# Attention and two MLPs on one core: the first matrix of each MLP by one level of Strassen, one MLP after the other

## The chip, the cores and the metric

The kernel runs on one core of a Trainium2 chip. The metric is the device time of one execution in microseconds (us). Three runs of the kernel before gave 1108.28, 1108.68 and 1110.57 us; the median is 1108.68.

## What is computed

All arrays are fp32. q, k and v are [1, 6016, 256].

```python
qn = q / (norm(q, axis=1) + 1e-6);  kn = k / (norm(k, axis=1) + 1e-6)
s = kn.transpose(0, 2, 1) @ qn / tau          # 256 x 256
a = softmax(s, axis=-1)
x = (v @ a).reshape(6016, 256)
h = x @ w_in                                  # 256 -> 2048, first MLP
x2 = (h * sigmoid(1.702 * h)) @ w_out         # 2048 -> 256
h = x2 @ w2_in                                # 256 -> 2048, second MLP
out = (maximum(h, 0) + alpha * minimum(h, 0)) @ w2_out
```

## The kernel before

Every fp32 product is made of three fp32r matmuls (`split_product`, L307 to L310): the high part of the weights by the high part of the data, high by low, and low by high. The high part is a rounded copy, which ScalarE writes; the low part is the fp32 value less the high one, which VectorE writes (L618), and at the start GpSimd too (L295 to L302).

The attention stage (to about 52 us) streams q and k, sums their squares, forms the 256 x 256 softmax, and folds it into the first matrix of the first MLP: W1P, eight pieces of 512 columns and six matmuls (L435 to L439). v then goes straight into the first MLP.

The MLPs work on the transposed data: features on partitions, tokens along the free axis. There are twelve token tiles, one of 384 tokens and eleven of 512, and for each a pass "A" (first MLP) and a pass "B" (second MLP). A pass has 16 chunks f of 128 hidden features. In each, `first_product` (L312) makes one bank of h from six matmuls, over two halves of 128 input features, and `second_product` (L333) adds six matmuls into two banks of output sums, two chunks later (LAG = 2). `phase_steps` (L352) writes this order out by hand; the passes go A0, A1, B0, A2, then nine turns of a hardware loop with B and A, then B10, B11. A whole tile is thus carried through both MLPs, and x2 never leaves the core.

Between the two matmul groups of a chunk stand, in "A", ScalarE's two activations out of PSUM (L474 to g, L477 to g_hi) and VectorE's low part (L618); in "B", two VectorE operations (L634 and L638, the leaky ReLU), ScalarE's rounding (L482) and the low part. v tiles come by DMA in blocks of 32 x 32 and are transposed by VectorE (L655), which also transposes the results (L680).

## Time and profile before

| | |
|---|---|
| median of 3 runs | 1108.68 us |
| span of the profiled execution | 1106.9 us |
| TensorE busy | 1098.3 us, 4937 matmuls |
| VectorE busy | 623.9 us, 954 instructions |
| ScalarE busy | 405.2 us, 715 instructions |
| GpSimd busy | 29.4 us, 28 instructions |
| granted clock of TensorE | 1.000 |

All times are of one profiled execution; its span is from the first to the last instruction, and the time of an execution holds a little before and after it. Matmuls are pipelined: one is shown with some 0.39 us, but the next starts 0.23 us later, so rates are read from start to start. "Idle before" names what released an engine after it had waited.

### The profile page before, as it was taken

How to read it: one execution, taken by the hardware profiler on the slowest of the kernel's cores; microseconds unless marked ns; L12 is line 12 of the kernel's file. 1: busy time of each engine (PE TensorE's matmuls, PEld its weight loads, DVE VectorE, ACT ScalarE, POOL GpSimd, SP SyncE). 2: the span in 40 equal slices, each digit the busy share in tenths (PEclk: the TensorE clock that was granted, in tenths of full speed). 3: DMA queues.
4: the chain of work that ended last, by engine and by line, in shares of the span. 5: the costliest groups of instructions: out<-in, count | busy, mean ns of one | idle time of the engine just before them, and what ended most of it. 6: DMA issues, size and time to landing. Idle time of an engine off the chain costs nothing.

```text
span 1106.9 us, 13843 instructions
## 1 busy us (share of the span) xinstructions
PE 1098.3 (99%) x4937; PEld 912.6 (82%) x4937; DVE 623.9 (56%) x954; ACT 405.2 (37%) x715; POOL 29.4 (3%) x28
## 2 busy tenths in 40 slices
PE   9999999999999999999999999999999999999998
PEld 8899898888888888888888888888888888888886
DVE  6974474275276257258348437527626725834775
ACT  6785523323323323322432432332332332343221
POOL 4500000000000000000000000000000000000000
PEclk9999999999999999999999999999999999999999
DMA  8742000010010110110100100001001011010011
GB/s 338 271 118 77 0 1 15 1 20 10 10 20 0 19 19 0 19 19 0 19 14 5 19 5 14 14 5 19 5 14 19 0 19 19 0 19 0 1 20 20
DMA packets 108536, 33.37 MB, mean 30 GB/s; under 512 B 100048, under 2 KB 104672, under 8 KB 108256
## 3 DMA queue, kind: packets, MB, share of 16 engines
q1 hardware_dynamic: 30368, 23.34, 6.7%
q10 hardware_dynamic: 78144, 9.71, 5.7%
q8 instruction: 15, 0.25, 0.1%
q14 instruction: 9, 0.07, 0.0%
HBM read 26.88 MB, written 6.16 MB: 30 GB/s over the span
## 4 chain that ended last, share of the span: by engine, by line
PE 98%; DMA 1%; DVE 0%; SPq 0%; ACT 0%; issue 0%
PE ps L308 32%; PE ps L309 32%; PE ps L310 32%; PE ps L401 2%; DMA q_sb<-q_dram 1%; PE ps L435 0%; PE ps L439 0%; PE ps L436 0%; DVE inv_norm L732 0%; SPq L259 0%; DVE sim L735 0%; SPq L260 0%; DVE neg_max L737 0%; DVE out_sb L680 0%; ACT sim L539 0%
## 5 line engine op out<-in xcount | busy, mean ns | idle before, releaser
L618 DVE TENSOR_TENSOR g_lo<-g,g_hi 128x512 fp32r<-128x512 f32 (+1 forms) x384 | 259.6, 676 | 341.0 <-ACT g_hi L477 331.2
L482 ACT ACTIVATE g_hi<-g 128x512 fp32r<-128x512 f32 (+1 forms) x192 | 119.7, 623 | 400.4 <-DVE g L638 400.4
L474 ACT ACTIVATE g<-ps 128x512 f32<-128x512 f32 (+1 forms) x192 | 113.1, 589 | 275.9 <-PE ps L310 275.9
L634 DVE TENSOR_SCALAR neg_part<-ps,alpha_T 128x512 f32<-128x512 f32 (+1 forms) x192 | 141.9, 739 | 125.4 <-PE ps L310 125.4
L308 PE MATMUL ps<-g_hi,w1o_hi 128*128 128x512 f32 (+1 forms) x384 | 150.1, 391 | 0.0
L309 PE MATMUL ps<-g_lo,w1o_hi 128*128 128x512 f32 (+1 forms) x384 | 150.1, 391 | 0.0
L310 PE MATMUL ps<-g_hi,w1o_lo 128*128 128x512 f32 (+1 forms) x384 | 150.0, 391 | 0.0
L308 PE MATMUL ps<-g_hi,w2o_hi 128*128 128x512 f32 (+1 forms) x384 | 148.0, 385 | 0.0
L309 PE MATMUL ps<-g_lo,w2o_hi 128*128 128x512 f32 (+1 forms) x384 | 147.9, 385 | 0.0
L310 PE MATMUL ps<-g_hi,w2o_lo 128*128 128x512 f32 (+1 forms) x384 | 147.9, 385 | 0.0
L308 PE MATMUL ps<-vT_hi,w1i_hi 128*128 128x512 f32 (+1 forms) x352 | 136.8, 389 | 0.0
L309 PE MATMUL ps<-vT_lo,w1i_hi 128*128 128x512 f32 (+1 forms) x352 | 136.7, 388 | 0.0
L310 PE MATMUL ps<-x_hi,w2i_lo 128*128 128x512 f32 (+1 forms) x352 | 135.5, 385 | 0.0
L310 PE MATMUL ps<-vT_hi,w1i_lo 128*128 128x512 f32 (+1 forms) x352 | 135.4, 385 | 0.0
L309 PE MATMUL ps<-x_lo,w2i_hi 128*128 128x512 f32 (+1 forms) x352 | 135.3, 384 | 0.0
L308 PE MATMUL ps<-x_hi,w2i_hi 128*128 128x512 f32 (+1 forms) x352 | 135.2, 384 | 0.0
L638 DVE SCALAR_TENSOR_TENSOR g<-ps,neg_part 128x512 f32<-128x512 f32 (+1 forms) x192 | 129.4, 674 | 0.4
L477 ACT ACTIVATE g_hi<-ps 128x512 fp32r<-128x512 f32 (+1 forms) x192 | 112.2, 584 | 0.0
L310 PEld LDWEIGHTS ps<-g_hi,w1o_lo 128*128 128x128 f32 x384 | 72.1, 188 | 16.1
L308 PEld LDWEIGHTS ps<-g_hi,w1o_hi 128*128 128x128 f32 x384 | 72.1, 188 | 15.7
L309 PEld LDWEIGHTS ps<-g_lo,w1o_hi 128*128 128x128 f32 x384 | 72.1, 188 | 15.2
L308 PEld LDWEIGHTS ps<-g_hi,w2o_hi 128*128 128x128 f32 x384 | 72.1, 188 | 14.6 <-DVE g_lo L618 0.4
(106 smaller groups left out, 1053.3 us busy)
## 6 DMA issues: line engine op xcount, KB each, us to landing
k_sb<-k_dram SPq DMA_DIRECT2D x10, 512.0 KB, 11.5
q_sb<-q_dram SPq DMA_DIRECT2D x10, 512.0 KB, 13.2
out_dram<-out_sb ACTq DMA_DIRECT2D x76, 64.0 KB, 1.9
v_raw<-v_dram ACTq DMA_DIRECT2D x72, 64.0 KB, 2.0
stage<-w_in_dram SPq DMA_DIRECT2D x4, 512.0 KB, 13.5
w1o_raw<-w_out_dram SPq DMA_DIRECT2D x1, 2048.0 KB, 8.6
stage<-w_in_dram SPq DMA_DIRECT2D x1, 2048.0 KB, 9.2
stage<-w_out_dram SPq DMA_DIRECT2D x1, 2048.0 KB, 8.3
```

The costliest lines, as they stand in the source:

```text
L308: nc.tensor.matmul(into, w_hi_ap, x_hi_ap, start=first, stop=False)
L309: nc.tensor.matmul(into, w_hi_ap, x_lo_ap, start=False, stop=False)
L310: return nc.tensor.matmul(into, w_lo_ap, x_hi_ap, start=False, stop=last)
L401: last = nc.tensor.matmul(ps[:, m, 0:C], k_sb[:, j, m * P:(m + 1) * P], q_sb[:, j, :], start=(j == 0), stop=False)
L474: nc.scalar.activation(g[:, f % 2, 0:n], ps[:, H + f % NH, 0:n], ACT.Gelu_apprx_sigmoid)
L477: nc.scalar.activation(g_hi[:, f % NG, 0:n], ps[:, H + f % NH, 0:n], ACT.Gelu_apprx_sigmoid).then_inc(hi_ready, 1)
L482: nc.scalar.activation(g_hi[:, f % NG, 0:n], g[:, f % 2, 0:n], ACT.Copy).then_inc(hi_ready, 1)
L618: return nc.vector.tensor_tensor(lo, full, hi.bitcast(fp32), ALU.subtract)
L634: nc.vector.tensor_scalar(neg_part[:, f % 2, 0:n], h, 0.0, alpha_T[:, f:f + 1], ALU.min, ALU.mult).then_inc(neg_done, 1)
L638: nc.vector.scalar_tensor_tensor(out=g[:, f % 2, 0:n], in0=h, scalar=0.0, in1=neg_part[:, f % 2, 0:n], op0=ALU.max, op1=ALU.add).then_inc( ...
```

## The change

The first product of each MLP is computed by the Winograd form of Strassen's scheme. A step n takes two token blocks (of 448 tokens in the first pair, of 512 in the other five) and two chunks of 128 hidden features, with two halves of the input features: a 2 x 2 by 2 x 2 block product, in seven products of three matmuls in place of eight. Weights and data enter as seven combinations each (`wi_hi`, `wi_lo`, `x_hi`, `x_lo`): four of them are sums, made by GpSimd (`wide_tops`, `wi_tops`, `tops_1` to `tops_4`; for the first two chunks of weights by VectorE). Products 1, 6, 7 and 4 add up in one bank, and ScalarE copies the bank to SBUF (`keep`) after each of the first three; VectorE's `sum_block` adds these copies to the banks of products 2, 5 and 3 and gives the blocks G11, G22 and G12; G21 is the bank itself. The second product of step n-1 is issued within step n, in four runs of six matmuls, in the order that `turn_order` gives, into four banks of sums.

A pair of blocks has 8 steps, an MLP has 48, and both have 96. The whole first MLP comes first; its result is copied out (`take_out`) and stored in a DRAM tensor, x2_stash, and loaded again for the second MLP, whose weights take the place of the first's during steps 41 to 52. The activations now read blocks of fp32 in SBUF (G21 from PSUM); in the second MLP ScalarE makes the negated part with ReLU, and VectorE adds it with the factor 1 - alpha (`leak`). All stores go by the queue of SP. The program has no hardware loops. The attention stage is as before, but all of W1P comes ahead of the first step, ScalarE alone takes it out of PSUM, and it is made into sums and split afterwards.

```diff
+    PAIRS = -(-N // (2 * W))
+    FIRST = (N - (PAIRS - 1) * 2 * W) // 2
+    QUADS = NF // 2
+    LAYER = PAIRS * QUADS
+    STEPS = 2 * LAYER
...
+        PRODUCT = {1: (0, 0), 2: (1, 5), 3: (6, 2), 4: (2, 6), 5: (3, 1), 6: (4, 3), 7: (5, 4)}
...
+        B11, T1, B22, T2, T3, B21, T4 = range(TOPS)
+        G11, G12, G21, G22 = range(4)
+        BLOCK = {G11: (0, 0), G12: (0, 1), G21: (1, 0), G22: (1, 1)}
...
+            return (G11, G21, G22, G12) if n % QUADS in (0, QUADS - 1) else (G11, G22, G21, G12)
...
+                if LAYER - QUADS <= n < LAYER:
+                    if s > 0:
+                        sp.wait_ge(wi_low, s)
+                    else:
+                        sp.wait_ge(wide_low, NFB - 1)
+                    for h in range(KC):
+                        sp.dma_start(wi_raw[:, 0:8:A21, :] if h == 0 else wi_raw[:, 1:3, :], w2i_v[h, s]).then_inc(wi_in, 16)
+                if LAYER - 4 <= n < LAYER - 4 + QUADS:
+                    s = n - (LAYER - 4)
+                    sp.wait_ge(wo_low, QUADS + s - 1)
+                    sp.dma_start(wo_raw[:, s % 2], w2o_v[s]).then_inc(wo_in[s % 2], 16)
...
+            for fb in range(NFB):
+                pool.wait_ge(w0_high, fb * KC + 2)
+                cols = slice(fb * BANK, (fb + 1) * BANK)
+                minus(w0_lo[:, 1, cols], stage[:, 1, cols], w0_hi[:, 1, cols].bitcast(fp32)).then_inc(w0_pool, 1)
+                if fb == 1:
+                    tops_1(0)
+                if fb == 2:
+                    tops_23(0)
+                    tops_4(0)
...
+            def wide_lows(fb):
+                pool.wait_ge(wide_high, fb + 1)
+                s = slice(2 * fb, 2 * fb + 2)
+                minus(wi_lo[:, s], wide[:, fb, :, 0:TOPS, :], wi_hi[:, s].bitcast(fp32)).then_inc(wide_low, 1)
+            wide_tops(1)
+            wide_lows(1)
...
+            def top(product, n, bank, first):
+                nt, s, gp = width(n), n % QUADS, pair(n)
+                w, x = PRODUCT[product]
+                if s == 0:
+                    pe.wait_ge(x_low, TOPS * gp + x + 1)
+                into = ps[:, bank, 0:nt]
+                xh, xl = x_hi[gp % 2][:, x, 0:nt], x_lo[gp % 2][:, x, 0:nt]
+                nc.tensor.matmul(into, wi_hi[:, s, w, :], xh, start=first, stop=False, skip_group_check=True)
+                nc.tensor.matmul(into, wi_hi[:, s, w, :], xl, start=False, stop=False, skip_group_check=True)
+                nc.tensor.matmul(into, wi_lo[:, s, w, :], xh, start=False, stop=True,
+                                 skip_group_check=True).then_inc(p_done[product], 1)
...
+            def second(n, begin, end):
...
+                order = turn_order(n)
+                for m in range(begin, end):
+                    b = order[m // 6]
+                    c, kind = divmod(m % 6, 3)
+                    i, t = BLOCK[b]
+                    f = 2 * s + i
+                    if m == 0 and n % LAYER < QUADS:
+                        pe.wait_ge(wo_low, layer(n) * QUADS + s + 1)
+                    if m % 6 == 0:
+                        pe.wait_ge(g_low[b], n + 1)
+                    opens = s == 0 and b in (G11, G22)
+                    if opens and kind == 0 and gp > 0:
+                        pe.wait_ge(y_out, 4 * (gp - 1) + 2 * t + c + 1)
+                    closes = s == QUADS - 1 and b in (G21, G12)
...
+                    done = nc.tensor.matmul(ps[:, 2 * t + c, 0:nt], wl if kind == 2 else wh, (g_lo if kind == 1 else g_hi)[:, b, 0:nt],
+                                            start=opens and kind == 0, stop=closes and kind == 2, skip_group_check=True)
+                    if m % 6 == 5:
+                        done.then_inc(y_used[b], 1)
+                    elif closes and m % 6 == 2:
+                        done.then_inc(y_half, 1)
...
+            def step(n):
+                if n < STEPS:
+                    if n >= 2:
+                        pe.wait_ge((acted if layer(n - 2) == 0 else leaky)[G21], n - 1 - LAYER * layer(n - 2))
...
+                    top(1, n, Y(n), True)
+                if n > 0:
+                    second(n - 1, 0, 6)
+                    pe.wait_ge(c_ready[G22], n)
+                    top(3, n - 1, Z, False)
+                if n < STEPS:
+                    pe.wait_ge(p1_kept, n + 1)
+                    top(6, n, Y(n), False)
+                if n > 0:
+                    second(n - 1, 6, 12)
+                if n < STEPS:
+                    if n > 0:
+                        pe.wait_ge(c_ready[G11], n)
+                    top(2, n, X, True)
+                    pe.wait_ge(u2_kept, n + 1)
+                    top(7, n, Y(n), False)
+                if n > 0:
+                    second(n - 1, 12, 18)
+                if n < STEPS:
+                    if n > 0:
+                        pe.wait_ge(c_ready[G12], n)
+                    top(5, n, Z, True)
+                    pe.wait_ge(u3_kept, n + 1)
+                    top(4, n, Y(n), False)
+                if n > 0:
+                    second(n - 1, 18, 24)
...
+            widen(0)
+            widen(1)
+            x_part(0, B11)
+            split_w0(3)
+            x_part(0, T1)
+            widen(2)
+            widen(3)
+            wide_part(0)
+            x_part(0, B22)
+            x_part(0, T2)
+            widen(4)
+            widen(5)
+            x_part(0, T3)
+            x_part(0, B21)
+            widen(6)
+            widen(7)
+            x_part(0, T4)
+            load_table(ACT.Gelu_apprx_sigmoid)
+            wo_part(0)
...
+            for n in range(STEPS + 1):
+                gp, s = pair(n) + 1, n % QUADS
+                if n < STEPS:
+                    keep(n, 0, 1, p1_kept)
+                if n > 0:
+                    high(n - 1, G21)
+                    activate(n - 1, G12)
+                if n < STEPS:
+                    keep(n, 1, 6, u2_kept)
+                if n > 0:
+                    high(n - 1, G12)
+                if n == STEPS:
+                    continue
+                if n in (0, 2, 3):
+                    wide_part({0: 1, 2: 2, 3: 3}[n])
+                if LAYER - 6 <= n < LAYER - 6 + QUADS:
+                    wi_part(n - (LAYER - 6))
...
+                activate(n, G11)
+                keep(n, 2, 7, u3_kept)
+                high(n, G11)
...
+                if LAYER - 3 <= n < LAYER - 3 + QUADS:
+                    wo_part(n + 3)
+                activate(n, G22)
+                activate(n, G21)
+                high(n, G22)
...
+            def sum_block(n, b):
...
+                product, bank, kept = {G11: (2, X, 0), G22: (5, Z, 2), G12: (3, Z, 1)}[b]
+                dve.wait_ge(p_done[product], n + 1)
+                dve.wait_ge({G11: p1_kept, G22: u3_kept, G12: u2_kept}[b], n + 1)
+                nc.vector.tensor_tensor(g[:, b, 0:nt], part[:, kept, 0:nt], ps[:, bank, 0:nt], ALU.add).then_inc(c_ready[b], 1)
...
+            for n in range(STEPS + 2):
+                gp, s = pair(n) + 1, n % QUADS
+                if s == 1 and n > 1:
+                    take_out(gp - 2, 1, 0)
+                    take_out(gp - 2, 1, 1)
+                if n == STEPS + 1:
+                    continue
+                if n > 0:
+                    low_block(n - 1, G22)
+                    sum_block(n - 1, G12)
+                    if layer(n - 1) == 1:
+                        low_block(n - 1, G21)
+                        leak(n - 1, G12)
+                    else:
+                        low_block(n - 1, G21)
+                if n < STEPS:
+                    sum_block(n, G11)
+                if n > 0:
+                    low_block(n - 1, G12)
+                if n < STEPS:
+                    if layer(n) == 1:
+                        leak(n, G11)
...
+                    if n < QUADS - 1:
...
+                    if LAYER - 3 <= n < LAYER - 3 + QUADS:
...
+                    sum_block(n, G22)
+                    low_block(n, G11)
...
+                    if layer(n) == 1:
+                        leak(n, G22)
+                        leak(n, G21)
+                if s == 0 and n > 0:
+                    take_out(gp - 2, 0, 0)
+                    take_out(gp - 2, 0, 1)
```

## Rows read from the trace of the kernel before

**Rows 1.** The page: busy shares, the chain; then whom TensorE waited for.
```profile
PE 1098.3 (99%) x4937; PEld 912.6 (82%) x4937; DVE 623.9 (56%) x954; ACT 405.2 (37%) x715; POOL 29.4 (3%) x28
...
PE 98%; DMA 1%; DVE 0%; SPq 0%; ACT 0%; issue 0%
...
PE ps L401 <- DMA q_sb<-q_dram: 1.6, 1, 1.6
PE ps L378 <- POOL ones L288: 1.1, 1, 1.1
PE ps L422 <- ACT sim L539: 0.8, 2, 0.4
```

**Rows 2.** The timeline of TensorE (start, us, operation) where passes begin.
```profile
138.99 0.33 PE L308 MATMUL ps<-x_hi,w2i_hi 128*128 128x384 f32 x1
...
173.05 0.39 PE L308 MATMUL ps<-vT_hi,w1i_hi 128*128 128x512 f32 x1
...
348.68 0.39 PE L308 MATMUL ps<-vT_hi,w1i_hi 128*128 128x512 f32 x1
...
393.19 0.39 PE L308 MATMUL ps<-x_hi,w2i_hi 128*128 128x512 f32 x1
...
436.84 0.39 PE L308 MATMUL ps<-vT_hi,w1i_hi 128*128 128x512 f32 x1
```

**Rows 3.** The timeline of single operations in steady passes, and one low part's wake.
```profile
501.64 0.39 PE L310 MATMUL ps<-x_hi,w2i_lo 128*128 128x512 f32 x1
502.07 0.75 DVE L634 TENSOR_SCALAR neg_part<-ps,alpha_T 128x512 f32<-128x512 f32 x1 [0.77 <-PE ps L310]
...
509.57 0.63 ACT L482 ACTIVATE g_hi<-g 128x512 fp32r<-128x512 f32 x1 [2.09 <-DVE g L638]
510.11 1.14 ACT L495 ACTIVATE vT_hi<-v_turn 128x512 fp32r<-128x512 f32 x2
...
1059.00 0.68 DVE L618 TENSOR_TENSOR g_lo<-g,g_hi 128x512 fp32r<-128x512 f32 x1
1059.60 0.68 DVE L638 SCALAR_TENSOR_TENSOR g<-ps,neg_part 128x512 f32<-128x512 f32 x1
...
1098.62 0.69 DVE L618 TENSOR_TENSOR g_lo<-g,g_hi 128x512 fp32r<-128x512 f32 x1 [0.70 <-ACT g_hi L482]
...
1099.37 0.50 PE L308 MATMUL ps<-g_hi,w2o_hi 128*128 128x512 f32 x1
```

**Rows 4.** The timeline of GpSimd and VectorE in the attention stage.
```profile
38.31 1.28 POOL L295 TENSOR_TENSOR w1o_lo<-k_sb,w1o_hi 128x512 fp32r<-128x512 f32 x1 [0.36 <-DVE w1o_hi L701]
39.28 1.21 DVE L708 TENSOR_TENSOR q_acc<-q_acc,ps 128x1024 f32<-128x1024 f32 x1
...
43.10 1.68 POOL L302 TENSOR_TENSOR w_lo<-stage,w_hi 128x512 fp32r<-128x512 f32 x1 [2.27 <-ACT w_hi L528]
43.57 1.49 DVE L714 TENSOR_TENSOR q_acc<-q_acc 128x256 f32<-128x256 f32 x1
44.98 0.41 DVE L714 TENSOR_TENSOR k_acc<-k_acc 128x256 f32<-128x256 f32 x1
...
53.60 1.30 POOL L302 TENSOR_TENSOR w_lo<-stage,w_hi 128x512 fp32r<-128x512 f32 x1 [2.84 <-ACT w_hi L528]
54.08 1.37 DVE L618 TENSOR_TENSOR w_lo<-stage,w_hi 128x512 fp32r<-128x512 f32 x1
```

**Rows 5.** The timeline where the first MLP begins, TensorE and ScalarE.
```profile
57.85 0.41 PE L308 MATMUL ps<-vT_hi,w1i_hi 128*128 128x384 f32 x1
...
58.63 1.28 ACT L499 ACT_TABLE_LOAD   x1
```

**Rows 6.** The end: last stores; then stretches with the granted clock (seventh column).
```profile
1101.12 2.25 SPq L249 DMA_DIRECT2D out_dram<-out_sb  x4
1101.13 2.35 ACTq L249 DMA_DIRECT2D out_dram<-out_sb  x4
...
1101.00:1104.00 3.00, 0.73 (x4) 0.25 (x2) 0.81 (x2) 0.00 (x0) 0.00 (x0) 1.00 0.66 90
1104.00:1106.00 2.00, 0.00 (x0) 0.00 (x0) 0.00 (x0) 0.00 (x0) 0.00 (x0) 0.94 0.93 127
1106.00:1107.00 1.00, 0.00 (x0) 0.00 (x0) 0.00 (x0) 0.00 (x0) 0.00 (x0) 0.50 0.00 0
```

More of the change, by code:

```diff
@@ new lines, in fixed @@
+        def fixed(name, shape, dt=fp32):
+            size = 4
+            for n in shape[1:]:
+                size *= n
+            made = place(name, shape, dt, base[0])
+            base[0] += -(-size // 32) * 32
+            return made
+        ident = fixed("ident", [P, P])
+        ones = fixed("ones", [P, P])
+        alpha_raw = fixed("alpha_raw", [NF, P])
+        alpha_T = fixed("alpha_T", [P, NF])
+        rest_T = fixed("rest_T", [P, NF])
+        tau_b = fixed("tau_b", [P, 1])
@@ L244, in move_out @@
[L244 to L252 removed]
+        NFB = FF // BANK
+        W1P = [(fb, m) for fb in range(NFB) for m in range(KC)]
@@ L286, in _ @@
+            store(sp, 2 * PAIRS - 1)
+            sp.wait_ge(stored, stored_by(2 * PAIRS))
         @block.gpsimd
@@ new lines, in leak @@
+            def leak(n, b):
+                nt = width(n)
+                f = 2 * (n % QUADS) + BLOCK[b][0]
+                dve.wait_ge(acted[b], n + 1)
+                nc.vector.scalar_tensor_tensor(out=g[:, b, 0:nt], in0=below[{G11: 1, G22: 0, G21: 1, G12: 0}[b]][:, 0:nt],
+                                               scalar=rest_T[:, f:f + 1], in1=ps[:, Y(n), 0:nt] if b == G21 else g[:, b, 0:nt],
+                                               op0=ALU.mult, op1=ALU.add).then_inc(leaky[b], 1)
```

846 lines of the change are left out of this document (405 added, 441 removed).

## The prediction

> **What bounds the kernel now.** I read the page's busy shares first, then the chain that ended last, then who TensorE waited for, then TensorE's timeline where one tile gives way to the next. TensorE is busy over 99% of the span, the chain is 98% TensorE, and its largest wait behind an operation is 1.6 us, once, for the first keys [rows 1]. So only two things can shorten this kernel: fewer or faster matmuls, or less lead-in and tail. VectorE (56%) and ScalarE (37%) have room on average, which says nothing yet about a single step.
> The rate comes from the tile boundaries. A 512-wide tile of the first MLP takes 192 matmuls from 348.68 to 393.19: 0.2318 us each. The second MLP's takes 192 from 393.19 to 436.84: 0.2273. The mean is 0.2296. The 384-wide tile runs from 138.99 to 173.05: 0.1774 [rows 2]. Three matmuls (0.69 us) are a product, and I write mm for one matmul of 0.23 us.
>
> **Part 1, fewer matmuls.** Now 22 tile passes of 192 at 0.2296 and two of 192 at 0.1774: 969.8 + 68.1 = 1037.9 us. The rewrite has 96 steps (6 pairs of token blocks, 8 steps each, two MLPs). A step is seven products for the first matrix (21 matmuls where eight products had 24) and the unchanged 24 for the second: 45. 80 steps are 512 wide: 3600 x 0.2296 = 826.6. 16 are 448 wide, and midway between 0.1774 and 0.2296 is 0.2035: 720 x 0.2035 = 146.5. Sum 973.1, so **-64.8 us**. At the rates 0.2273 or 0.2318 for the wide ones it moves by 8.3 either way; nothing in the trace says which of the two the new operands will have.
> The Trainium skill ("TensorE: Matmul & The Clock Gate", Back-to-back issue gap) gives columns / 2.4 plus 2.5 ns, 215.7 ns at 512 columns. The rows show 227 to 232. By the page the 4320 matmuls would take about 913 us instead of 973; the rows decide, and the sum stays.
>
> **Part 2, what each step now waits for.** A step in order, at 0.23 us each, with n-1 the step before: product 1 (0 to 0.69), run 1 of six second-product matmuls of n-1 (to 2.07), product 3 of n-1 (to 2.76), product 6 (to 3.45), run 2 (to 4.83), products 2 and 7 (to 6.21), run 3 (to 7.59), products 5 and 4 (to 8.97), run 4 (to 10.35). A result is there for VectorE 0.43 us after its last matmul starts, which is 0.2 after the end in this count. A VectorE pass over 512 columns takes 0.68 and the next starts after about 0.6, a ScalarE copy 0.63 with 0.55 between starts, and TensorE follows VectorE after 0.07 [rows 3].
> ScalarE: 11 passes a step (3 keeps, 4 activations, 4 roundings), 6.1 us of 10.35. VectorE: 7 in the first MLP, 11 in the second, 6.7 us. Both fit. The kept sums come in time: keep of product 1 from 0.89 to 1.5, wanted at 2.76; of product 6 from 4.3 to 4.9, wanted at 5.52; of product 7 from 7.0 to 7.6, wanted at 8.28.
> One does not. Block G12 of n-1 is summed on VectorE after product 3: 2.96 to 3.64. The low part of G21 stands behind that sum in VectorE's queue: 3.57 to 4.25, so TensorE may use it at 4.32. In six of eight steps G21 is the third run (6.21) and nothing is late. But turn_order puts it second for the first and the last step of a pair, and there run 2 wants it at 3.45: **0.87 us idle**. That is at steps with n mod 8 = 0 and 1: 23 times (the 24th is in the tail): **+20.0**. What is queued behind the wait is all of TensorE.
> In the second MLP, at the end of the first step of a pair, VectorE has sum G22, low G11, two leaks and only then the two copies out of the banks, whose first ends at 11.8. The next step's run 1 opens that bank and wants it at 11.04: 0.8 us, five times, **+4.0**.
>
> **Part 3, GpSimd and VectorE.** The first MLP's Strassen sums of weights and inputs go to GpSimd, which is idle after the start now. A subtraction of 512 columns takes it 1.28 us, 2.5 ns a column [rows 4]. I count 5376 + 3072 columns (first weights), 7168 + 4096 (second weights) and 24,600 (inputs): 44,300 columns or 111 us. When such an operation overlaps one of VectorE's with both inputs in SBUF, one waits for the other: a 256-column addition took 1.49 us where its twin took 0.41 (GpSimd was busy from 43.10 to 44.78), the low part at 54.08 took 1.37 instead of 0.68, while accumulations that read PSUM kept 1.21 beside it [rows 4]. All low parts of the new kernel are of the first kind.
> The Trainium skill ("SBUF — State Buffer", Who interferes with whom) speaks against the change here: it calls this an exclusive lock for the whole instruction on VectorE's second read port, taken with two SBUF inputs. By that, a 1792-column subtraction shuts VectorE's low parts out for its whole length; if it were shared bandwidth instead, the terms below would be about half. The rows lean to the lock.
> In the steps of a pair with x sums, six pairs per MLP, most such blocks end inside slack (low G11 is ready 1.3 us before it is wanted); the second MLP's steps 3 and 4 lose perhaps 0.5 each. **+5**, bounds 0 and 15.
>
> **Part 4, the start.** Now the first MLP product begins at 57.85 [rows 5] with half of the folded weights still to come: 24 matmuls x 0.23 = 5.6, so 63.4 us of lead-in. In the rewrite all eight pieces of W1P come first, and nothing is interleaved. W1P's last two wait for w0_pool, which GpSimd gives only after four input sums that in turn wait for low parts from VectorE: about 63.4 if no operation is held up, 69 if each waits its turn. Two more pieces (2.8), then on ScalarE two widenings, one rounding, the table load (1.28, [rows 5]) and wo_part stand ahead of the first keep: product 6 of step 0 at 70.4 or 75.8. Step 0 has nothing else to do while ScalarE keeps three sums: it ends 5 us later, at 75.4 or 80.9, less 4.3 for its own 21 matmuls: lead-in 71 to 76.6, so +8 to +13. Then come three 1792-column subtractions (4.5 us each) ahead of low parts that steps 1, 3 and 4 wait for: 0 to 2.9 us each. I take **+17** for all, bounds +9 and +26.
>
> **Part 5, between the two MLPs and at the end.** In steps 42 to 49 the second MLP's weights are loaded, summed on GpSimd, rounded on ScalarE and subtracted on GpSimd (896 columns, 2.3 us), and SP's queue puts the load for wo_part behind a wait for wi_low. At steps 47 and 48 that load goes out at about 9.0 and lands near 12, where ScalarE wants it at 9: about 2 us each, and a few tenths in the other steps. **+7**, bounds 2 and 12. At the end run 2 waits 1.6 us for G21 with no products beside it, and the last half is stored by SP alone, four issues of 0.4 where SP and ScalarE have two each now [rows 6]: **+2.5**, bounds 1 and 4. The x2 round trip (3 MB through HBM) is loaded most of a pair ahead, and the longer unrolled program is like the unrolled first 260 us of now, where TensorE waits for nothing behind the attention [rows 1]: 0 each.
>
> **Sum.** -64.8 + 20.0 + 4.0 + 5 + 17 + 7 + 2.5 = -9.3. The profiled span is 1106.9 [rows 1]; it becomes 1097.6. The median of the runs lies 1.8 above that span, so the forecast is **1099.4 us**.
>
> **Rivals.** (a) *GpSimd becomes what VectorE, and through it TensorE, waits for.* Slower. The place is every low part that stands on a short chain; the price is the share of 111 us of GpSimd time that reaches TensorE. The forecast has some 5 us of it in the pairs, and about 8 in start and transition. It decides from 9.3 us more, one fifth of the total instead of an eighth. At one third it is 24 us more: 1123; a middle value is **1115**. For it: rows 4, and the second MLP's VectorE at two thirds full. Against it: most input sums run where nothing is due.
> (b) *Slack swallows most waits.* Start at its bound (-8), transition and pairs at theirs (-10), and the rate 0.2273 (-8): **1073**. For it: neither engine is full, and a wait in one place leaves slack in the next. Against it: the 0.87 us follows from queue order alone.
> (c) *TensorE's clock falls in the start.* The granted clock is 1.00 after a wait of 1.6 us, but 0.94 and then 0.50 in the slices after the last matmul [rows 6]. The start of the rewrite has two waits of 3 to 6 us. At half clock a matmul costs 0.2 us more; 20 to 40 of them are 4 to 8 us: **1105**. The Trainium skill ("TensorE: Matmul & The Clock Gate", What you observe) has the same two levels and would put it down to idleness; rows show it only at the end.
> That the count of products does not fall is excluded by the code (seven calls of top with three matmuls each).
>
> **How the numbers follow.** Forecast 0.50 (its own range 1088 to 1112), (a) 0.28, (b) 0.14, (c) 0.08. A measurement of this kernel tells 0.2% (2.2 us) from no change. Faster: 0.42 + 0.14 + 0.03 = 0.59. Same: 0.05 + 0.02 + 0.01 = 0.08. Slower: 0.03 + 0.26 + 0.04 = 0.33. Range 1076 to 1122: it leaves out the low end of (b) and the high end of (a), with the far tails of the rest.
>
> **What would show it.** The count of matmuls must fall by 288 at about 0.23 us apart inside a run. TensorE's waits must name the low part of G21 at 0.9 us, once in every first and second step of a pair, and none elsewhere but at the start and in steps 42 to 49. The first step should begin near 66 to 72 and the ninth some 12 us behind its matmuls. VectorE's low parts should show means above 0.69 wherever GpSimd runs. If idle time of TensorE in a middle pair of the first MLP is over 4 us, a chain that I called short is not; if it is zero, queue order does not bind as I read it.

## The result and the profile after

The changed kernel takes 1136.55 us (median of four runs, 1135.38 to 1138.55) where the kernel before takes 1108.63: a ratio of 1.0249 (95% interval 1.0234 to 1.0263). The forecast was 1099.4 with a range up to 1122. It is 28 us slower, and 37 us from the forecast.

The page of the kernel after answers [rows 1]:

```profile
span 1133.9 us, 13268 instructions
...
PE 1056.4 (93%) x4649; PEld 873.7 (77%) x4649; DVE 752.2 (66%) x1100; ACT 689.2 (61%) x1235; POOL 158.6 (14%) x131
...
PE   9959899999999999998976899999999999999996
...
PEclk9988999999999999999888999999999999999999
...
PE 78%; DVE 7%; issue 4%; ACT 4%; POOL 3%; DMA 2%; SPq 1%; ACTq 0%; POOLq 0%; DVEq 0%
```

The 288 matmuls are gone (4937 to 4649). TensorE is no longer alone on the chain of work that ended last: 98% became 78%. The two rows by slices, each slice 28 us, say where: TensorE drops in the third and fifth slice and again in slices 19 and 21 to 23, and the granted clock drops in slices 3 and 4 and in 20 to 22. Before, one wait of 1.6 us was the largest. After, the view of waits reads (engine and line, releaser: total, times, longest):

```profile
PE ps L433 <- DVE g_lo L753: 40.6, 37, 3.9
PE ps L433 <- DVE out_sb L883: 9.9, 6, 5.4
PE ps L410 <- ACT part L555: 8.5, 4, 4.2
PE ps L537 <- issue: 6.5, 1, 6.5
```

Most of the 37 waits for g_lo, the short ones at the two ends of a pair, were forecast; the long ones were not. All the rest follows from reading three stretches apart.

**A steady pair.** TensorE's timeline in the first MLP, then at the two ends of a pair in the second (answers [rows 2]). A row that closes with brackets is one that TensorE waited for; the time in brackets is some 0.15 us less than the delay from start to start.

```profile
343.72 0.50 PE L433 MATMUL ps<-g_hi,wo_hi 128*128 128x512 f32 x1 [0.70 <-DVE g_lo L753]
...
345.23 0.39 PE L410 MATMUL ps<-x_hi,wi_hi 128*128 128x512 f32 x1
...
355.45 0.39 PE L410 MATMUL ps<-x_hi,wi_hi 128*128 128x512 f32 x1
...
427.36 0.50 PE L433 MATMUL ps<-g_hi,wo_hi 128*128 128x512 f32 x1 [0.70 <-DVE g_lo L753]
...
790.56 0.47 PE L433 MATMUL ps<-g_hi,wo_hi 128*128 128x512 f32 x1 [0.89 <-DVE out_sb L883]
...
866.75 0.50 PE L433 MATMUL ps<-g_hi,wo_hi 128*128 128x512 f32 x1 [0.70 <-DVE g_lo L753]
...
951.65 0.50 PE L433 MATMUL ps<-g_hi,wo_hi 128*128 128x512 f32 x1 [0.70 <-DVE g_lo L753]
```

An undisturbed step takes 355.45 - 345.23 = 10.22 us, or 0.2271 a matmul. Eight of them are 81.8, and the pair took 427.36 - 343.72 = 83.64: the 1.9 beyond are the two waits for the low part of G21 (0.86 each, by which the matmul starts late, and 0.1 more since the next one follows it after 0.34 instead of 0.23) and nothing else. In the second MLP a pair took 84.90, with the wait for out_sb (1.05) beside the two.

**The start.** TensorE, GpSimd, VectorE and ScalarE in order of time, answers [rows 4, 5]:

```profile
55.49 1.52 DVE L839 TENSOR_TENSOR wide<-wide 128x256 f32<-128x256 f32 x1
...
58.97 5.77 POOL L308 TENSOR_TENSOR x_raw<-x_raw 128x448 f32<-128x448 f32 x3 [2.24 <-DVE x_lo L753]
64.70 1.64 POOL L308 TENSOR_TENSOR w_lo<-stage,w_hi 128x512 fp32r<-128x512 f32 x1
...
66.44 0.77 PE L537 MATMUL ps<-w_hi,attn_T_hi 128*128 128x512 f32 x1 [6.51 <-issue]
67.00 0.63 PE L538 MATMUL ps<-w_lo,attn_T_hi 128*128 128x512 f32 x1
...
71.70 0.39 PE L410 MATMUL ps<-x_hi,wi_hi 128*128 128x448 f32 x1
...
79.32 4.00 POOL L308 TENSOR_TENSOR wi_lo<-wide,wi_hi 128x1792 fp32r<-128x1792 f32 x1 [8.95 <-ACT wi_hi L555]
...
81.16 2.70 DVE L753 TENSOR_TENSOR wo_lo<-wo_raw,wo_hi 128x512 fp32r<-128x512 f32 x1 [2.31 <-ACT wo_hi L555]
...
85.07 0.45 PE L433 MATMUL ps<-g_hi,wo_hi 128*128 128x448 f32 x1 [3.39 <-DVE g_lo L753]
```

W1P's seventh piece waits 6.5 us for one low part that GpSimd makes behind three input sums. Its matmuls are then 0.43 us apart, not 0.23. At 81.16 a low part of VectorE takes 2.70 us in place of 0.69, while GpSimd's 1792-column subtraction runs until 83.32; behind it in VectorE's queue stand a sum and the low part that TensorE waits for.

**Between the MLPs.** The chain of one step, from the view of the chain (start, us, what), and the matmul at its end:

```profile
561.27 0.85 ACT wi_hi L555
...
562.19 2.13 POOL wi_lo L308
...
564.34 0.38 SPq L286
...
564.76 0.47 SPq L286
...
565.27 2.83 DMA wo_raw<-w_out_dram
...
568.13 0.64 ACT wo_hi L555
...
568.79 0.04 DVE wo_lo L753
...
569.40 0.68 DVE g L858
570.08 0.61 DVE g_lo L753
...
570.73 1.65 PE ps L433 x3
```

SP's load of the next wo_raw stands behind two loads that wait for GpSimd's wi_lo; ScalarE waits 3.56 us for it and rounds it to wo_hi. VectorE waits for wo_hi, because in its queue the low part of these weights (wo_lo) stands ahead of the sum and of the low part (g_lo) that TensorE needs. The same repeats at 587 and 603, and at 621 the wait is for a copy of VectorE. The stretches of these waits show a clock near the half (us, then each engine; the seventh column is the granted clock, 1.00 being 2.4 GHz; the first row is a steady stretch):

```profile
200.00:210.00 10.00, 10.00 (x46) 8.29 (x45) 6.40 (x9) 7.04 (x13) 1.29 (x1) 1.00 0.18 28
570.00:577.00 7.00, 6.27 (x15) 4.91 (x16) 3.73 (x7) 3.94 (x8) 0.00 (x0) 0.51 0.00 0
```

15 matmuls stand in 7 us from 570, where 30 fit. In the stretches where the granted clock is 0.50, one matmul starts 0.37 to 0.43 us after the last in place of 0.20 to 0.23. Summed over them this is about 8 us of matmul time at the start (49 matmuls) and 10 between the MLPs (54). Elsewhere the clock is full up to the last matmul.

### The profile page after: what moved, and what is told of

Read it like the earlier page. It is cut to its first block, busy times and chain, and to the rows that moved or that the text cites. A ratio compares the mean times of both kernels' runs of the same rounds, so it can differ in the third digit from the quotient of the medians.

```text
span 1133.9 us, 13268 instructions
## 1 busy us (share of the span) xinstructions
PE 1056.4 (93%) x4649; PEld 873.7 (77%) x4649; DVE 752.2 (66%) x1100; ACT 689.2 (61%) x1235; POOL 158.6 (14%) x131
## 4 chain that ended last, share of the span: by engine, by line
PE 78%; DVE 7%; issue 4%; ACT 4%; POOL 3%; DMA 2%; SPq 1%; ACTq 0%; POOLq 0%; DVEq 0%
PE ps L433 41%; PE ps L410 11%; PE ps L412 11%; PE ps L411 11%; DVE g L858 3%; DVE g_lo L753 2%; PE ps L503 2%; POOL wi_lo L308 2%; DVE g L865 1%; DMA wo_raw<-w_out_dram 1%; ACT wo_hi L555 1%; ACT wi_hi L555 1%; ACT g_hi L555 1%; DMA q_sb<-q_dram 1%; DMA wi_raw<-w_in_dram 1%
## 5 line engine op out<-in xcount | busy, mean ns | idle before, releaser
L858 DVE TENSOR_TENSOR g<-part,ps 128x512 f32<-128x512 f32 (+1 forms) x288 | 194.6, 676 | 286.0 <-PE ps L412 278.3
L433 PE MATMUL ps<-g_hi,wo_hi 128*128 128x512 f32 (+1 forms) x768 | 303.7, 395 | 50.5 <-DVE g_lo L753 40.6
L433 PE MATMUL ps<-g_lo,wo_hi 128*128 128x512 f32 (+1 forms) x768 | 299.5, 390 | 0.0
L433 PE MATMUL ps<-g_hi,wo_lo 128*128 128x512 f32 (+1 forms) x768 | 299.2, 390 | 0.0
L410 PE MATMUL ps<-x_hi,wi_hi 128*128 128x512 f32 (+1 forms) x672 | 263.9, 393 | 8.8 <-ACT part L555 8.5
L411 PE MATMUL ps<-x_lo,wi_hi 128*128 128x512 f32 (+1 forms) x672 | 262.1, 390 | 0.0
L412 PE MATMUL ps<-x_hi,wi_lo 128*128 128x512 f32 (+1 forms) x672 | 261.7, 389 | 0.0
L555 ACT ACTIVATE part<-ps 128x512 f32<-128x512 f32 (+1 forms) x288 | 165.6, 575 | 17.8 <-PE ps L412 17.8
L433 PEld LDWEIGHTS ps<-g_hi,wo_lo 128*128 128x128 f32 x768 | 146.2, 190 | 27.9
L433 PEld LDWEIGHTS ps<-g_lo,wo_hi 128*128 128x128 f32 x768 | 146.2, 190 | 26.3
```

What stands on the lines that cost most here:

```text
L410: nc.tensor.matmul(into, wi_hi[:, s, w, :], xh, start=first, stop=False, skip_group_check=True)
L411: nc.tensor.matmul(into, wi_hi[:, s, w, :], xl, start=False, stop=False, skip_group_check=True)
L412: nc.tensor.matmul(into, wi_lo[:, s, w, :], xh, start=False, stop=True, skip_group_check=True).then_inc(p_done[product], 1)
L433: done = nc.tensor.matmul(ps[:, 2 * t + c, 0:nt], wl if kind == 2 else wh, (g_lo if kind == 1 else g_hi)[:, b, 0:nt], start=opens and kind ...
L555: return nc.scalar.activation(into, of, ACT.Copy)
L858: nc.vector.tensor_tensor(g[:, b, 0:nt], part[:, kept, 0:nt], ps[:, bank, 0:nt], ALU.add).then_inc(c_ready[b], 1)
```

## The experiments

Each kernel is the changed one with the edit shown. Differences are between the ratios to the kernel before (1108.6 to 1109.9 us in these comparisons), times 1109; the ratio of the changed kernel is 1.0249 +- 0.0015, so a difference is good to some 2.5 us. The +1.8 of e3_pieces and the -2.1 of e10_warm are not clear of zero.

| kernel | median us | ratio to before, 95% | against the changed kernel |
|---|---|---|---|
| e1_order | 1115.47 | 1.0066 (1.0044 to 1.0089) | -20.3 |
| e2_queue | 1116.18 | 1.0055 (1.0036 to 1.0074) | -21.5 |
| e3_pieces | 1139.92 | 1.0265 (1.0244 to 1.0286) | +1.8 |
| e4_nowi | 1107.06 | 0.9971 (0.9960 to 0.9983) | -30.8 |
| e5_warm | 1153.10 | 1.0404 (1.0387 to 1.0422) | +17.2 |
| e6_w0first | 1131.33 | 1.0196 (1.0174 to 1.0219) | -5.9 |
| e7_wifirst | 1111.60 | 1.0025 (1.0015 to 1.0035) | -24.8 |
| e8_all | 1068.23 | 0.9639 (0.9623 to 0.9655) | -67.6 |
| e9_lows | 1120.70 | 1.0108 (1.0093 to 1.0124) | -15.6 |
| e10_warm | 1134.13 | 1.0230 (1.0216 to 1.0244) | -2.1 |
| e11_best | 1065.78 | 0.9608 (0.9595 to 0.9621) | -71.1 |
| e12_takeout | 1131.82 | 1.0206 (1.0192 to 1.0220) | -4.8 |

### Is it the order of the runs? e1_order

```diff
-            return (G11, G21, G22, G12) if n % QUADS in (0, QUADS - 1) else (G11, G22, G21, G12)
+            return (G11, G22, G21, G12)
```

> The changed kernel with one order of the four runs in every step (G11, G22, G21, G12), where it had G21 second in the first and last step of a pair. Queue order theory: TensorE waits 0.86 us for the low part of G21 in 23 steps, because that low part stands behind the sum of G12 on VectorE; with G21 third all these waits go and nothing is late in their place: 1136.5 - 23 x 0.86 = 1117 us, and a first-MLP pair takes 81.9 us instead of 83.6. Rival, VectorE's load: the copies out of the banks and the low parts come later anyway, and the wait moves to G22 or to the copies: 1130 to 1136.

The waits for G21 at the ends of the pairs are gone, and the last one, in the tail, fell from 1.54 to 0.72. The time fell by 20, and in the pairs no other wait took their place; between the MLPs the wait for out_sb grew from 5.4 to 6.7 us. So the mechanism behind the +20.0 is shown. That the size agrees to 0.3 us is in part luck: by the starts of the steps, each of 18 steps is 1.00 us shorter (11.20 became 10.20), not 0.87, and the waits in 448-wide steps were shorter than 0.86.

### SP's queue between the MLPs: e2_queue

```diff
+                if LAYER - 4 <= n < LAYER - 4 + QUADS:
+                    r = n - (LAYER - 4)
+                    sp.wait_ge(wo_low, QUADS + r - 1)
+                    sp.dma_start(wo_raw[:, r % 2], w2o_v[r]).then_inc(wo_in[r % 2], 16)
                 if LAYER - QUADS <= n < LAYER:
...
-                if LAYER - 4 <= n < LAYER - 4 + QUADS:
-                    s = n - (LAYER - 4)
-                    sp.wait_ge(wo_low, QUADS + s - 1)
-                    sp.dma_start(wo_raw[:, s % 2], w2o_v[s]).then_inc(wo_in[s % 2], 16)
```

> The changed kernel with SP's load of a second-MLP wo_raw piece put ahead of the wait for wi_low in the same step, where it stood behind it. Queue theory: in steps 45 to 48 ScalarE waited 3.6, 3.2, 4.3 and 2.5 us for wo_raw, and each time TensorE then idled some 4 us and fell to half clock. With the load a step earlier these waits go, and TensorE's loss in steps 45 to 48 (25 us) falls to under 8: 1117 to 1121 us. Rival, round trip of the weights: the chain ScalarE, GpSimd, SP, DMA, GpSimd for wi_raw takes over a step, so ScalarE waits there instead and the kernel stays above 1130.

Two loads swapped in one queue give 21.5 us. Of the four waits of 3.5, 3.2, 3.9 and 5.4 us between 570 and 621 two are gone and two became 0.9 and 2.6:

```profile
542.02 0.73 PE L410 MATMUL ps<-x_hi,wi_hi 128*128 128x512 f32 x1 [4.07 <-ACT part L555]
555.59 0.50 PE L410 MATMUL ps<-x_hi,wi_hi 128*128 128x512 f32 x1 [1.50 <-ACT part L555]
...
603.62 0.71 PE L433 MATMUL ps<-g_hi,wo_hi 128*128 128x448 f32 x1 [2.62 <-DVE out_sb L883]
```

The first two rows have another cause, since they stay: ScalarE there waits for GpSimd.

### GpSimd's queue ahead of them: e7_wifirst

On top of e2_queue, GpSimd does the weights of the second MLP ahead of the input sums of the same step.

```diff
+                if LAYER - 6 <= n < LAYER - 6 + QUADS:
+                    wi_lows(n - (LAYER - 6))
+                if LAYER - 7 <= n < LAYER - 7 + QUADS:
+                    wi_tops(n - (LAYER - 7))
                 if gp < 2 * PAIRS and s == 1:
                     tops_1(gp)
...
-                if LAYER - 6 <= n < LAYER - 6 + QUADS:
-                    wi_lows(n - (LAYER - 6))
-                if LAYER - 7 <= n < LAYER - 7 + QUADS:
-                    wi_tops(n - (LAYER - 7))
```

> The kernel with SP's wo_raw load put ahead of the wait for wi_low, and also GpSimd's second-MLP weight work put ahead of the input sums in each step. In the kernel with the first edit alone TensorE still waited 4.2 and 1.7 us at steps 43 and 44, where two input sums (2.7 us) stood ahead of the subtraction for wi_low on GpSimd. Queue order theory: these waits go, and the half clock behind the first: 1116.2 - 7 = 1109 us. Rival, round trip too long in itself (ScalarE, GpSimd 2.1, DMA 3.8, GpSimd 1.8 us): the wait stays near 3 us and it comes to 1113 to 1116.

3.3 us less than e2_queue by the ratios (4.6 by the medians), about half of the 7 expected. Both waits for part, 4.07 and 1.50, are gone. In the kernel after, the first of them was two input sums of 1.35 us each in front of the wi_lo that ScalarE's next rounding hung on:

```profile
528.22 2.71 POOL L308 TENSOR_TENSOR x_raw<-x_raw 128x448 f32<-128x448 f32 x2 [33.71 <-DVE x_lo L753]
530.90 2.13 POOL L308 TENSOR_TENSOR wi_lo<-wi_raw,wi_hi 128x896 fp32r<-128x896 f32 x1
...
538.65 0.95 ACT L555 ACTIVATE wi_hi<-wi_raw 128x896 fp32r<-128x896 f32 x1 [5.28 <-POOL wi_raw L308]
```

### What that whole stage costs: e4_nowi

The edit takes out the loads of wi_raw, `wi_tops`, `wi_part` and `wi_lows` with their waits, so this kernel leaves out the second MLP's first weights and its result is another one.

> Leaves out loading, summing, rounding and subtracting the second MLP's first weights (it goes on with the first MLP's); all matmuls stay, and the wo weights are still exchanged. Chain theory: steps 43 to 49 lose their 36 us but for the regular 0.9 us waits, because wo_raw's load no longer stands behind a wait for wi_low: 1136.5 - 36 = 1100 us, and TensorE holds full clock there. Rival: the exchange of wo weights by itself (a load in each step into two buffers) costs half of it: 1115 to 1120.

30.8 us less, where the theory expected 36. So of the 39 us of the transition (below), 31 hang on the second MLP's first weights, and e7_wifirst gets 24.8 of them back with the same work done.

### Is it the shared port? e3_pieces

```diff
-                minus(wi_lo[:, s], wide[:, fb, :, 0:TOPS, :], wi_hi[:, s].bitcast(fp32)).then_inc(wide_low, 1)
+                for x in range(TOPS):
+                    last = minus(wi_lo[:, s, x], wide[:, fb, :, x, :], wi_hi[:, s, x].bitcast(fp32))
+                last.then_inc(wide_low, 1)
```

and the same for wi_lows, in pieces of 128 columns.

> The changed kernel with GpSimd's subtractions of 1792 and 896 columns cut into seven each, by product; the same work, shorter instructions. Lock theory (VectorE's operations with two SBUF inputs wait for the whole GpSimd instruction): low parts of VectorE that took 2.7 and 2.8 us in steps 0 and 2 take under 1.5, TensorE's waits before 85.1, 108.2 and 122.6 us shrink by 1 to 2 each, and likewise a little in steps 42 to 49: 1128 to 1132 us. Rival, shared bandwidth: cutting changes nothing for VectorE, and GpSimd gets longer by its fixed cost: 1136 to 1142.

The rival's number came, and GpSimd did get longer by its fixed cost. But VectorE's low part got short, as the lock theory says; GpSimd and VectorE, where the kernel after had 4.00 and 2.70 us:

```profile
80.06 6.10 POOL L308 TENSOR_TENSOR wi_lo<-wide,wi_hi 128x256 fp32r<-128x256 f32 x7 [7.70 <-ACT wi_hi L559]
...
81.90 0.82 DVE L757 TENSOR_TENSOR wo_lo<-wo_raw,wo_hi 128x512 fp32r<-128x512 f32 x1 [2.81 <-ACT wo_hi L559]
```

VectorE was held up by one short piece, not by the sum of seven: 0.82 us. What it gained was paid by GpSimd, whose seven pieces take 6.10 us where one instruction took 4.00, and whatever waited for wi_lo came 2 us later: waits of 4.9, 5.9 and 7.1 us between the MLPs. The experiment has two effects of opposite sign and can't price the lock.

### The low parts given to VectorE: e9_lows

```diff
-            wide_lows(1)
...
+            def wide_lows(fb):
+                dve.wait_ge(wide_high, fb + 1)
+                s = slice(2 * fb, 2 * fb + 2)
+                low(wi_lo[:, s], wide[:, fb, :, 0:TOPS, :], wi_hi[:, s]).then_inc(wide_low, 1)
+
+            def wi_lows(s):
+                dve.wait_ge(wi_high, s + 1)
+                low(wi_lo[:, s], wi_raw[:, 0:TOPS, :], wi_hi[:, s]).then_inc(wi_low, 1)
...
+                    if n in (0, 2, 3):
+                        wide_lows({0: 1, 2: 2, 3: 3}[n])
+                    if LAYER - 6 <= n < LAYER - 6 + QUADS:
+                        wi_lows(n - (LAYER - 6))
```

> The changed kernel, with one edit: the low parts of the Strassen weights (three blocks of 1792 columns in steps 0, 2 and 3, eight of 896 columns in steps 42 to 49) are subtracted by VectorE between its other passes, and GpSimd keeps only the sums. Theory (the two engines shut each other out, and what is queued behind a shut-out pass comes late): the passes beside a sum of GpSimd no longer stretch from 0.69 to 2.7 us, the block before step 4 is ready earlier, and the wait for a round trip between ScalarE, GpSimd and SP in the transition loses 2.1 us a step at GpSimd against about 1 us more of VectorE: 8 to 15 us less, 1122 to 1129 us. Rival (the work is on the chain whoever does it, and VectorE is now the late one): within 4 us of the changed kernel, 1133 to 1140 us, with waits of TensorE for g_lo in the same steps.

15.6 us less, just beyond the 8 to 15 that the theory gave. The edit does two things at once (no long GpSimd instruction beside VectorE, and a shorter way to wi_lo; GpSimd's wi_tops gets a wait for wi_low with it), and the run doesn't separate them. VectorE does 1792 columns in half of GpSimd's time, and the wo_lo behind it takes 0.68 again. The last row is the wait that the kernel after has at 122.60, so 7.2 us of the gain lie ahead of it:

```profile
79.13 2.03 DVE L741 TENSOR_TENSOR wi_lo<-wide,wi_hi 128x1792 fp32r<-128x1792 f32 x1 [0.42 <-ACT wi_hi L543]
81.08 0.68 DVE L741 TENSOR_TENSOR wo_lo<-wo_raw,wo_hi 128x512 fp32r<-128x512 f32 x1
...
115.40 0.61 PE L421 MATMUL ps<-g_hi,wo_hi 128*128 128x448 f32 x1 [1.95 <-DVE g_lo L741]
```

### The start: e6_w0first

```diff
                 if fb == 1:
                     tops_1(0)
-                if fb == 2:
-                    tops_23(0)
-                    tops_4(0)
+            tops_23(0)
+            tops_4(0)
```

> The changed kernel with GpSimd's last low part of w0 ahead of three of the four input sums of the first pair, where it stood behind them. Queue order theory: the seventh and eighth piece of W1P start near 60 us instead of 66.4, ScalarE reaches the first keep at 68 to 70 instead of 75.0, and TensorE keeps its full clock: 1128 to 1131 us. Rival: the input sums are then the last to come, since they share the port with VectorE's low parts, and step 0 waits for them just as long: 1134 to 1137.

From start to start W1P's wait fell from 6.67 to 0.81 us, and its last twelve matmuls run 0.23 apart, which is 2.4 us more. The time fell by 5.9 all the same: a new wait of 1.5 us, for wi_lo, stands before step 0, the wait of 3.2 for ScalarE's first copy stays, and against the expectation the clock falls there (0.50 from 67.9 to 74.7).

### The clock: e5_warm and e10_warm

Matmuls of the constant `ones` (`keep_clock`, which the attention stage already uses) fill TensorE's waits. In e5_warm:

```diff
+                if i == 6:
+                    keep_clock(100)
...
                     top(1, n, Y(n), True)
+                    if n == 0:
+                        keep_clock(45)
```

> The changed kernel with 100 small matmuls of ones on ones ahead of the wait for the seventh piece of W1P, and 45 more between products 1 and 6 of step 0: TensorE is given work while it waits. In the changed kernel the granted clock reads 0.74 from 60 to 80 us and single matmuls follow each other at 0.37 to 0.43 us instead of 0.20 to 0.23. Clock theory: 12 matmuls of W1P and some 10 of step 0 come 0.2 us sooner each, 3 to 4.5 us in all: 1132 to 1133.5. Rival, the slow spacing is only the trace of waits and does not add: 1136 to 1137, or later by what the extra matmuls overhang.

The sizing was mistaken: a call is two records of 0.11 us, so 100 calls took 22.5 us and overhung the wait by some 16, the second batch by 7. The kernel is slower by about what they overhung less 6, and says only that W1P's last two pieces ran at 0.23 us behind them. e10_warm has the batches at the size of the waits, 27 and 13 calls.

> The changed kernel, with idle matmuls of 128 columns between the sixth and seventh pieces of W1P (27 calls, 6.1 us by 0.225 a call, in a wait of 6.67) and after product 1 of step 0 (13 calls, 2.9 us, in a wait of 3.25). They are sized to end before what TensorE waits for is there. Theory (after these waits TensorE runs at half clock, and that is time lost): the 12 matmuls of W1P's last two pieces start 0.23 apart in place of 0.43, and those of step 0 0.20 in place of 0.37; 3 to 5 us less, 1131.5 to 1133.5 us. Rival (what follows is bound by the other engines' chain, and the slow matmuls lie in its shadow): 1135.5 to 1137 us, with the waits longer by what the matmuls save. In steps 1 and 42 to 49 nothing changes under either.

TensorE at the same operations as above (66.44 to 71.70 after, now 66.89 to 69.72):

```profile
66.89 0.47 PE L541 MATMUL ps<-w_hi,attn_T_hi 128*128 128x512 f32 x1 [0.53 <-issue]
67.19 0.39 PE L542 MATMUL ps<-w_lo,attn_T_hi 128*128 128x512 f32 x1
...
69.72 0.36 PE L410 MATMUL ps<-x_hi,wi_hi 128*128 128x448 f32 x1
...
73.59 0.47 PE L410 MATMUL ps<-x_hi,wi_hi 128*128 128x448 f32 x1 [0.20 <-ACT part L559]
...
82.48 0.71 PE L433 MATMUL ps<-g_hi,wo_hi 128*128 128x448 f32 x1 [3.39 <-DVE g_lo L757]
```

Step 0 begins 2.0 us earlier, product 6 too (75.58 to 73.59), run 1 is 2.6 earlier (85.07 to 82.48); the medians differ by 2.4 us and the profiled spans by 3.7. At the start 21 matmuls run at half clock here and 49 in the kernel after, 4.9 us of matmul time less, and the end comes 2 to 4 us earlier. So a part of the slow matmuls was on the path; where the next thing to come is a ScalarE copy, faster matmuls turn into a longer wait (1.00 at 77.58 in place of 0.55 at 80.19). The result lies between the two expectations, nearer to the theory in the trace; the intervals of the two ratios overlap (a difference of 2.1 +- 2.3 us), so by the times alone the gain isn't shown.

### The copy out: e12_takeout

```diff
+                    if s == 0 and n > 0:
+                        take_out(gp - 2, 0, 0)
+                        take_out(gp - 2, 0, 1)
                     if layer(n) == 1:
                         leak(n, G22)
                         leak(n, G21)
...
-                if s == 0 and n > 0:
+                if n == STEPS:
```

> The changed kernel, with one edit: in the first step of a pair VectorE takes the first two banks of output sums out ahead of the two leaky operations, not after them. Theory (run 1 of the next step waited for these copies): the 1.05 us waits behind out_sb in the second MLP go, 5 x 1.05 = 5.3, and perhaps 1 of the 5.5 us wait behind out_sb between the MLPs; 1130 to 1132 us. Rival (the leaks, now later, delay the low parts of G22 and G21 by the same time, and TensorE waits for those instead): 1136 us, with waits behind g_lo in the same steps.

4.8 us less, and both theories have a share: all waits for out_sb but one are gone, while the wait for g_lo in the same step grew from 0.70 to 1.26 us at 706.62 and to 1.43 in the later pairs. By the starts of the steps the five pairs gain only 2.3 us together; the rest comes from the transition, where the wait for out_sb fell from 5.4 to 4.1.

### All together: e8_all and e11_best

e8_all has the edits of e1, e2, e6, e9 and e12, and `wi_tops` ahead of the input sums.

> The changed kernel with all that the theory names: one order of runs (-20), SP's load ahead of the wait (-20), GpSimd's last low part of w0 first (-6), weight sums before input sums on GpSimd (-6), the low parts of the Strassen weights on VectorE instead of GpSimd (no instruction of 2 to 4 us on the shared port any more, and a shorter round trip: -8), copies out of the banks ahead of two leaks (-5). If the terms add: 1136.5 - 65 = 1071 us, range 1064 to 1082, faster than the kernel before. Rival, they overlap, or VectorE's added passes (2.1 and 1.1 us each) come late on their own: 1085 to 1100.

It takes 1068.23 us, 3.6% less than the kernel before. The single effects nearly add up: 20.3 + 21.5 + 5.9 + 3.3 + 15.6 + 4.8 = 71.4 against 67.6 measured. Its page and its longest wait:

```profile
PE 1035.8 (97%) x4649; PEld 864.5 (81%) x4649; DVE 756.1 (71%) x1111; ACT 688.7 (65%) x1235; POOL 131.8 (12%) x120
...
PE 85%; DVE 8%; ACT 3%; issue 2%; DMA 1%; POOL 0%; SPq 0%; DVEq 0%; ACTq 0%; POOLq 0%
...
PE ps L397 <- ACT part L542: 3.9, 2, 3.2
```

e11_best adds to it the table load ahead of ScalarE's last x_hi, and 13 calls of keep_clock after product 1 of step 0.

> The kernel of e8_all, with ScalarE's table load put ahead of the last rounding of the first inputs (where ScalarE waited 0.57 us), and 13 calls of idle 128-column matmuls after product 1 of step 0 (2.9 us in a wait of 3.4). After that wait e8_all ran 16 matmuls at about 0.37 in place of 0.20, 2.7 us. Theory (clock on the path): 1.5 to 3 us less than e8_all's 1068.2, so 1065 to 1067 us. Rival (the steps after it are bound by ScalarE's and VectorE's chain): 1068 us.

1065.78 us, 3.9% less than before, and the fastest here. The medians are 2.4 us apart and the intervals of the ratios lie side by side (0.9595 to 0.9621, 0.9623 to 0.9655). In the profiled executions the path from the softmax (50.85 and 51.87) to the last wait for g_lo (1054.24 and 1055.17) is 1003.4 and 1003.3 us, the same: the half clock came later and for fewer matmuls (14 in place of 25), and the time didn't change. But the profiled execution is the slowest of e11_best's five. Its granted clock was 0.992 on average, and it took 1067.92 us; the others had 0.994, 0.996, 0.996 and 0.997 and took 1066.90, 1065.78, 1065.50 and 1064.93. The four of e8_all had 0.992, 0.991, 0.991 and 0.989 and took 1066.99, 1068.26, 1068.20 and 1070.45. So the time goes with the clock from one execution to the next, which speaks for the clock as the cause of the 2.4 us; no run has the table load alone, so its share isn't shown. In its profiled execution e8_all has it after the wait at 69.59, e11_best after the waits at 75.05 and 78.24 (granted clock in the seventh column, e8_all first):

```profile
71.00:74.00 3.00, 3.00 (x10) 2.48 (x8) 2.59 (x4) 2.88 (x4) 2.92 (x4) 0.50 0.14 24
...
77.00:80.00 3.00, 2.12 (x11) 2.01 (x12) 1.52 (x4) 2.38 (x5) 2.92 (x4) 1.00 0.03 5
```

```profile
75.00:80.00 5.00, 3.24 (x11) 2.66 (x12) 3.73 (x5) 3.36 (x7) 4.92 (x5) 0.65 0.12 41
```

## Why the prediction was wrong, step by step

| term | predicted | found | from |
|---|---|---|---|
| fewer matmuls | -64.8 | -64.8 | 288 fewer |
| their rate | 0 | about -9 | 0.2271 in place of 0.2296 at 512 columns, 0.2034 as forecast at 448 |
| G21's order | +20.0 | +20.3 | e1_order |
| copy out in the second MLP | +4.0 | +5.3 | 5 x 1.05 in the trace |
| GpSimd beside VectorE in the pairs | +5 | about 0 | 83.64 against 81.8 + 1.9; in e1_order all eight steps of a middle pair take 10.20 |
| start | +17 (9 to 26) | about +31 | up to 8 of it clock |
| between the MLPs | +7 (2 to 12) | about +39 | up to 10 of it clock |
| end | +2.5 (1 to 4) | about +5 | a wait of 1.54, and 3.6 more behind the last matmul |

The start: from 71.70, product 1 of step 0, to product 3 of step 7 at 163.63 pass 91.9 us for 342 matmuls of 448 columns, 69.6 at 0.2034. The 22.3 too many and the 71.70 make a lead-in of 94.0 where the kernel before has 63.4. Between the MLPs: from 530.13 to 635.83 pass 105.7 us for 315 matmuls, 243 of 512 columns and 72 of 448, which is 69.8. That is 35.9 too many; steps 50 to 53 lose 4.5 more behind it, and 1.3 of it all is counted as G21's order. The end: from the start of the last matmul to the end of the span pass 9.2 us, where it was 5.6. SP alone issues sixteen stores there, where before SP and ScalarE had four each [rows 6]:

```profile
1123.50 8.53 SPq L243 DMA_DIRECT2D out_dram<-out_sb  x16
```

The sum of what was found is about 27 us, against the 27.9 measured; each of the two large terms is good to 1 or 2 us.

**Right.** Part 2 reads one step as a timetable of queues, and its numbers held: 0.87 us forecast and 0.86 found, once in every first and second step of a pair of 512-wide blocks; 0.8 and 1.05 for the copy out. The claim that a middle pair has under 4 us of idle time holds as well. One sign of the prediction did not: waits of 0.7 to 1.5 us for g_lo stand also in steps 50 to 53, and it had said none there. The rate was slightly better than the mean of the two rates in [rows 2]; it lay at the lower one. The store and reload of x2 cost TensorE no wait, as forecast, though it is 6 MB each way and not 3.

**Wrong, the transition (part 5).** This term carries 32 of the 37 us. The prediction saw the very chain, with SP's load of wo_raw behind a wait for wi_low, and put it at "about 2 us each" in steps 47 and 48 and a few tenths elsewhere. TensorE waited 3.2 to 3.9 us in each of three steps and 5.4 in a fourth. The chain begins and ends in one queue, ScalarE's. From the start of wi_hi (561.17; the chain enters it at 561.27) to the landing at 568.10 it takes 6.9 us; in ScalarE's own queue wo_hi is wanted 3.4 us after wi_hi (568.13 less the wait of 3.56, less 561.17). The difference is paid in every step that has both, steps 45 to 48 (ScalarE waited 3.6, 3.2, 4.3 and 2.5 us), and can't be worked off: both ends move with ScalarE, so a late step doesn't bring the load any nearer. The step that failed is that the prediction dated the load from the step's nominal start ("at about 9.0") and let only steps 47 and 48 pay. Second, "a few tenths" missed the two input sums on GpSimd's queue ahead of wi_lo (a wait of 4.24 at 540.66). e2_queue and e7_wifirst give the two back by swaps of order alone, 21.5 and 3.3 us.

**Wrong, the clock, named only as a rival.** Rival (c) gave 4 to 8 us, at the start alone, and 8 in 100. The rate after a long wait belonged in the sum, for the prediction itself forecast waits of 3 to 6 us. Found: about 8 us of matmul time at the start and 10 in the transition. After each of TensorE's waits of 2.26 us and more in this kernel, 8 to 15 matmuls ran at half of 2.4 GHz; after those of up to 1.5 none did. It isn't all loss: e10_warm took away 4.9 us of it and got 2 to 4. The Trainium skill ("TensorE: Matmul & The Clock Gate", What you observe and What's actually happening) lays the two levels to how busy the engine has been; e10_warm agrees, where the same matmuls ran at 0.23 us once the wait ahead of them was filled.

**Half right, the start (part 4).** Single times held: W1P's seventh piece was forecast at 63.4 to 69 and came at 66.44, product 6 of step 0 at 70.4 or 75.8 and came at 75.58, step 0 ended at 80.9 as the later of its two dates said. Three low parts were to cost 0 to 2.9 us each; TensorE's waits for them were 3.4, 2.3 and 3.5. So each choice fell at its late end or just beyond, where the prediction took the middle. By its own parts the prediction could reach 13 + 8.7, some 22 us; its bound of 26 has no term behind it. Of the 31 found, 13 are there at the end of step 0 (with the half clock of W1P and step 0 in them), the three waits are 9.6 from start to start, the half clock behind them is 4.7, and the rest, 3 to 4, is in smaller waits.

**The rival (a)**, GpSimd as the wait, was the right kind of loss: e9_lows gains 15.6 us by taking 30 of the 159 us of GpSimd's time away, e6_w0first 5.9 by its order. But its place was wrong. In the pairs, where some 60 us of GpSimd's work lie, it cost nothing. At start and transition the length of the round trip seems to weigh more than VectorE's blocked passes, since cutting the subtraction in pieces (e3_pieces) gained nothing; no run has the two apart. The Trainium skill ("SBUF — State Buffer", Who interferes with whom) calls the shared port an exclusive lock for a whole instruction; the trace agrees (2.70 us beside a subtraction of 4.00, 0.82 beside pieces of 0.87), but what the lock costs depends on who is due behind the blocked pass, and in a steady pair nobody is.

What stays open: how much of the transition's 10 us of half clock was on the path, since no run filled those waits, how e9_lows divides between the port and the shorter trip, and a microsecond or two of the sum.

## What to carry to other kernels

Lay out queue order as a timetable, and where a wait leads back to its own engine over others (ScalarE, GpSimd, SP, a DMA, ScalarE), compare the length of that trip with the distance of its two ends in the queue: the difference is paid each time. Order in a queue was worth more than work here: swapping two loads on SP gave 21 us and one line of turn_order 20, of the 68 to 71 us by which the same arithmetic became faster. A wait of TensorE of about 2 us or more should carry in the sum the slow matmuls that may follow it. At the end, count the stores that one queue has to issue.

## What the runs showed of the hardware

- In these runs the granted clock fell to half during or just after all of TensorE's waits of 3 us and longer but two (3.10 at 76.06 in e1_order and at 76.94 in e3_pieces, with 1.00 behind them), and it stayed full with all of up to 1.5. Between them it went either way: at half after 1.95 us (e8_all at 109.35, e9_lows at 115.40), at full after 1.94 (e11_best at 112.06) and after 2.74 (e7_wifirst at 597.83). In e11_best two waits of 1.71 us, 3.2 us apart, were followed by half clock. After a wait of 2.26 (108.22 in the kernel after) the first five matmuls ran at full clock and those from 109.33 at half. The same kernel differs from one execution to the next: 0.972 to 0.977 on average in the kernel after, the lowest with the longest time (1138.55 us).
- Seven GpSimd subtractions of 256 columns take 6.10 us, one of 1792 columns 4.00, and VectorE's of 1792 columns 2.03. By these numbers (2.10 us for six more instructions) splitting work on GpSimd costs about 0.35 us for each further one.
- A VectorE pass that met a GpSimd subtraction took 2.70 in place of 0.69; beside short pieces 0.82.
- A fp32 matmul call of 128 columns is two records of 0.11 us.
